# Attention in front of two expert layers: inputs laid out channel-major on the host, u products on TensorE, a new order of the attention loop

## What is computed

```python
batch, n_heads, seq, head_dim = (2, 8, 768, 48)
for t in range(S):
    kt, vt, rt, wt = (k[:, :, t], v[:, :, t], r[:, :, t], w[:, :, t])
    cur = np.einsum('bhd,bhe->bhde', u[None] * kt, vt)
    y[:, :, t] = np.einsum('bhd,bhde->bhe', rt, state + cur)
    state = wt[:, :, :, None] * state + np.einsum('bhd,bhe->bhde', kt, vt)
```

## Time and profile before

| | us |
|---|---|
| median of 3 runs | 1204.25 (1198.97 to 1204.97) |
| the profiled execution | 1201.32 |
| span of its profile | 1199.6 |
| TensorE busy | 1161.1 (97% of the span) |
| VectorE busy | 504.4 (42%) |
| ScalarE busy | 448.9 (37%) |
| GpSimd busy | 243.8 (20%) |

### The profile page before, as it was taken

One profiled execution on the slowest core, in us unless ns is written; L12 is line 12 of the kernel. 1 busy time (PEld: TensorE's weight loads), 2 busy tenths in 40 slices (PEclk: granted clock), 3 DMA queues, 4 the chain that ended last, 5 costly groups with the idle time before them and its releaser, 6 DMA issues. The chain is left out here.

```text
span 1199.6 us, 18556 instructions
## 1 busy us (share of the span) xinstructions
PE 1161.1 (97%) x6968; PEld 1039.6 (87%) x6968; DVE 504.4 (42%) x949; ACT 448.9 (37%) x926; POOL 243.8 (20%) x247
## 2 busy tenths in 40 slices
PE   6999989999999999999999999999999998999997
PEld 4888769899999998999999899999999986999997
DVE  5777556222222222212222222212222353999996
ACT  4565352212212211221221122122123473888884
POOL 5544262202201210220221121022012210000001
PEclk9888799999999999999999999999999999999999
DMA  9741043040050031005005002200300303999991
GB/s 187 144 70 31 2 149 124 26 160 1 1 186 1 1 132 55 1 2 185 1 1 185 1 1 91 94 1 1 105 1 1 132 35 114 392 358 368 359 361 59
DMA packets 106982, 123.41 MB, mean 103 GB/s; under 512 B 52745, under 2 KB 95406, under 8 KB 106912
## 3 DMA queue, kind: packets, MB, share of 16 engines
q1 hardware_dynamic: 104928, 117.65, 31.1%
q0 software_dynamic: 1984, 4.75, 1.0%
HBM read 98.37 MB, written 25.39 MB: 103 GB/s over the span
## 5 line engine op out<-in xcount | busy, mean ns | idle before, releaser
L973 DVE SCALAR_TENSOR_TENSOR h_lo<-hid,h_hi 128x512 fp32r<-128x512 f32 x168 | 116.1, 691 | 497.8 <-ACT h_hi L836 497.8
L836 ACT ACTIVATE h_hi<-hid 128x512 fp32r<-128x512 f32 x168 | 100.5, 598 | 547.7 <-PE hid L1131 547.7
L794 POOL TENSOR_TENSOR w_lo<-raw,w_hi 128x384 fp32r<-128x384 f32 x128 | 130.8, 1022 | 644.2 <-ACT w_hi L828 644.2
L1144 PE MATMUL acc<-w_hi,h_hi 128*128 128x384 f32 x736 | 249.6, 339 | 0.0
L1144 PE MATMUL acc<-w_hi,h_lo 128*128 128x384 f32 x736 | 249.3, 339 | 0.0
L1144 PE MATMUL acc<-w_lo,h_hi 128*128 128x384 f32 x736 | 248.6, 338 | 0.0
L1131 PE MATMUL hid<-x_hi,w_hi 128*128 128x512 f32 x576 | 227.9, 396 | 0.5 <-issue 0.4
L1131 PE MATMUL hid<-x_hi,w_lo 128*128 128x512 f32 x576 | 227.6, 395 | 0.0
L1131 PE MATMUL hid<-x_lo,w_hi 128*128 128x512 f32 x576 | 227.3, 395 | 0.0
L1144 PEld LDWEIGHTS acc<-w_lo,h_hi 128*128 128x128 f32 x736 | 138.1, 188 | 8.6
L1144 PEld LDWEIGHTS acc<-w_hi,h_hi 128*128 128x128 f32 x736 | 138.1, 188 | 7.7
(11 more groups left out here) (255 smaller groups left out, 1464.1 us busy)
## 6 DMA issues: line engine op xcount, KB each, us to landing
raw<-in_moe_w SPq DMA_DIRECT2D x54, 1536.0 KB, 9.2
rows<-filler SPq DMA_DIRECT2D x8, 2328.0 KB, 16.4
m_x<-rows SPq DMA_DIRECT2D x19, 194.0 KB, 4.6
spread_w<-in_w SPq DMA_DIRECT2D x16, 144.0 KB, 4.2
spread_r<-in_r SPq DMA_DIRECT2D x16, 144.0 KB, 4.1
spread_k<-in_k SPq DMA_DIRECT2D x16, 144.0 KB, 4.3
v_sb<-in_v SPq DMA_DIRECT2D x16, 144.0 KB, 4.2
out_y<-m_y,m_token POOLq DMA_INDIRECT x19, 6.7
```

The lines of the kernel that those rows point to most:

```text
L794: pool.tensor_tensor(lo[q][m][:, a:b], raw[m][:, a:b], hi[q][m][:, a:b].bitcast(F32), ALU.subtract).then_inc(s_wlo, 1)
L836: act.activation(h_hi[st % HB][:, :], hid[st % HB][:, :], ACT.Relu).then_inc(s_hhi, 1)
L973: dve.scalar_tensor_tensor(h_lo[st % HB][:, :], hid[st % HB][:, :], 0.0, h_hi[st % HB][:, :].bitcast(F32), ALU.max, ALU.subtract).then_inc ...
L1144: mm = pe.matmul(acc[j][:, 0:DM], a[st % HB][:, j * P:(j + 1) * P], b[q][1][:, f * DM:(f + 1) * DM], start=(f == 0 and x == 0), stop=(f == ...
```

## The change

r, k and w are laid out by the host (`laid_out`) as the channel-major tiles that the kernel used to make, with zeros (ones for w) in the padding, and v as v_sb holds it. So `spread`, the turn-ins and ScalarE's three copies go; `w_pad`, `k_ch` and `r_ch` are loaded directly, a DMA each (128 rows of 3 KB), v with one DMA too, and u as 96 columns of which two are not zero (`u_cols`).

The u term is one GpSimd product `rk` of 768 columns, then six TensorE products of `rk` with the 96 columns of `u_cols` (`sums`), and a small ScalarE copy to `cur`, which has two buffers. Behind the scores, `sums(j+1)` stands ahead of out_tiles(j,0) in TensorE's order. The copy and four state steps become one scan over all tiles (`carry` holds the factors, made by ScalarE in `carries`; increments are written with a stride of 5). Each score half has its own PSUM banks. The identity products are 240 columns wide, one ahead of turn_back and one between the score halves (four at the end as before).

The orders are new. VectorE: pre and suf of i+1, states(i), outputs(i-1,1), masked(i,0), products and keys of i+1, masked(i,1), receivers(i+1), outputs(i,0). The memsets of `state_diag` come behind the first two scans, and TensorE's first instructions wait for them.

```diff
+FIRST, BACK, MIDDLE, LAST = 5, 1, 1, 4
+WIDE = 96
...
             for i in range(PAIRS):
-                q = i % 2
-                for n in "wrk":
-                    if i >= 2:
-                        sp.wait_ge(s_turn[n], i - 1)
-                        if n != "w":
-                            sp.wait_ge(s_rk, i - 1)
-                    for h in two:
-                        sp.dma_start(spread[n][q][:, :, h, 0:D], src[n][i, h]).then_inc(s_in[n][q], 16)
+                if i >= 2:
+                    sp.wait_ge(s_suf, i - 1)
+                load(w_pad, w, "w", i)
+                if i >= 2:
+                    sp.wait_ge(s_kblk, i - 1)
+                    sp.wait_ge(s_rk, i - 1)
+                load(k_ch, k, "k", i)
+                if i >= 2:
+                    sp.wait_ge(s_rblk, i - 1)
+                load(r_ch, r, "r", i)
...
+            receiver_keys(0)
+            for j in range(PAIRS):
+                scaled(j)
+                if j + 1 < PAIRS:
+                    receiver_keys(j + 1)
+                current_values(j)
...
+            current(0)
+            for j in range(PAIRS):
+                divided(j, 0)
+                if j == 0:
+                    act.wait_ge(d_init, 6)
+                carries(j)
+                rows(j)
+                halves(j)
+                divided(j, 1)
+                diagonal(j)
+                if j + 1 < PAIRS:
+                    current(j + 1)
...
+                dve.tensor_tensor_scan(state[q][:, :, :].rearrange("p d t -> p (d t)"), carry[q][:, :, :].rearrange("p d t -> p (d t)"),
+                                       turn[:, 0:(NT - 1) * D], 0.0, ALU.mult, ALU.add).then_inc(s_state, 1)
...
+                if ahead:
+                    before_block(i + 1)
+                if ahead:
+                    behind_block(i + 1)
...
+                if back:
+                    states(i)
+                if i >= 1:
+                    outputs(i - 1, 1)
                 if back:
                     masked(i, 0)
                 if ahead:
-                    behind_block(i + 1)
                     products(i + 1)
                     keys(i + 1)
...
+            def sums(j):
+                pe.wait_ge(s_rk, j + 1)
+                if j == 0:
+                    pe.wait_ge(s_u, 16)
+                for t in range(NT):
+                    mm = pe.matmul(turn[:, CUR + 2 * t:CUR + 2 * t + WIDE], rk[:, t * P:(t + 1) * P], u_cols[:, j % (H // 2), :],
+                                   start=True, stop=True, skip_group_check=True)
+                mm.then_inc(s_sums, 1)
...
+            pe.wait_ge(d_init, 6)
+            for g in range(G):
+                for h in two:
+                    pe.matmul(score[g][h][:, 0:TG * P], ident[:, :], state_diag[0][:, 0:TG, :, :].rearrange("p n h c -> p (n h c)"),
+                              start=True, stop=True, skip_group_check=True)
+            sums(0)
+            for j in range(PAIRS):
+                pe.wait_ge(s_cur, j + 1)
+                keep_clock(FIRST if j == 0 else BACK)
+                turn_back(j)
+                if j >= 1:
+                    out_tiles(j - 1, 1)
+                increments(j)
+                scores(j, 0)
+                keep_clock(MIDDLE)
+                scores(j, 1)
+                if j + 1 < PAIRS:
+                    sums(j + 1)
+                out_tiles(j, 0)
+            keep_clock(LAST)
+            out_tiles(PAIRS - 1, 1)
```

More of the change, by code:

```diff
@@ L89, in attention @@
         k_rows = sb("k_rows", [P, NT, P])
-        state = [sb(f"state{q}", [P, NT, D]) for q in two]
+        state = [sb(f"state{q}", [P, D, NT - 1]) for q in two]
         state_diag = [sb(f"state_diag{q}", [P, NT, 2, 64]) for q in two]
-        rku = sb("rku", [P, NT, 2, D])
-        cur = sb("cur", [P, NT, 2])
+        carry = [sb(f"carry{q}", [P, D, NT - 1]) for q in two]
+        rk = sb("rk", [P, S])
+        cur = [sb(f"cur{q}", [P, NT, 2]) for q in two]
         cur_v = sb("cur_v", [P, NT, 2, D])
         scores_sb = [[sb(f"scores_sb{g}{h}", [P, TG, P]) for h in two] for g in range(G)]
-        turn_a = ps("turn_a", [P, 1024])
-        turn_b = ps("turn_b", [P, 1024])
-        score = [ps(f"score{h}", [P, 512]) for h in two]
+        turn = ps("turn", [P, 1024])
+        CUR, IDLE = S, S + 16
+        score = [[ps(f"score{g}{h}", [P, 512]) for h in two] for g in range(G)]
         yps = [ps(f"yps{g}", [P, 512]) for g in range(G)]
@@ L166, in _ @@
         def _(pool):
[L167 to L172, removed]
             def coef(c, at):
@@ L262, in rows, with halves @@
                     act.wait_ge(s_inc, j)
-                act.activation(flat(k_rows), turn_b[:, 0:S], ACT.Copy).then_inc(s_rows, 1)
-                divided(j, 1)
+                act.activation(flat(k_rows), turn[:, 0:S], ACT.Copy).then_inc(s_rows, 1)
+            def halves(j):
+                q = j % 2
+                act.wait_ge(s_rblk, j + 1)
+                if j >= 2:
+                    act.wait_ge(s_score, 4 * (j - 1))
+                act.activation(pairs_of(kr_half[q], BLK, HALF + BLK, 64), pairs_of(kr_blk[q], BLK, S + BLK, P), ACT.Copy).then_inc(s_half_a, 1)
             def diagonal(i):
@@ L271, in diagonal, with carries, current @@
                     act.activation(state_diag[i % 2][64 * h:64 * h + 64, 1:NT, h, 0:D],
[L272 to L282, removed]
+                                   state[i % 2][64 * h:64 * h + 64, :, :].rearrange("p d t -> p t d"), ACT.Copy).then_inc(s_diag, 1)
+            def carries(j):
+                act.wait_ge(s_kblk, j + 1)
+                if j >= 2:
+                    act.wait_ge(s_state, j - 1)
+                act.activation(carry[j % 2][:, :, 1:NT - 1], coef_r[:, 1:NT - 1, BT].unsqueeze(1).broadcast_to([P, D, NT - 2]),
+                               ACT.Copy).then_inc(s_carry, 1)
+            def current(j):
+                act.wait_ge(s_sums, j + 1)
+                if j >= 2:
+                    act.wait_ge(s_curv, j - 1)
+                act.activation(flat(cur[j % 2][:, :, :]), turn[:, CUR:CUR + NT * 2], ACT.Copy).then_inc(s_cur, 1)
+            current(0)
[10 more added lines that the diff above has]
+                    current(j + 1)
         @block.vector
@@ L386, in _ @@
                 back, ahead = i >= 0, i + 1 < PAIRS
+                if ahead:
+                    before_block(i + 1)
+                if ahead:
+                    behind_block(i + 1)
+                if i == -1:
+                    for q in two:
+                        dve.memset(carry[q][:, :, :], 0.0)
+                    for q in two:
+                        diag = dve.memset(state_diag[q][:, :, :, :], 0.0)
+                    diag.then_inc(d_init, 1)
                 if back:
                     states(i)
-                if ahead:
-                    before_block(i + 1)
+                if i >= 1:
+                    outputs(i - 1, 1)
                 if back:
@@ L440, in turn_back @@
                 for t in range(NT):
-                    mm = pe.transpose(turn_b[:, t * P:(t + 1) * P], k_tile[:, t * P:(t + 1) * P], ident[:, :])
+                    mm = pe.transpose(turn[:, t * P:(t + 1) * P], k_tile[:, t * P:(t + 1) * P], ident[:, :])
                 mm.then_inc(s_back, 1)
```

203 lines of the change are left out of this document (60 added, 143 removed).

## The result

The changed kernel takes 1172.48 us (median of four, 1169.51 to 1173.07), the kernel before 1201.61 beside it. The ratio is 0.976, with an interval of 0.973 to 0.980. Executions over 1.5% above the fastest of their kernel are left out of every ratio here, and are named where they occur. I had forecast 1179.5 in a range of 1170 to 1196: the time lies in the range, 7 us under the forecast and on the first rival (full clock, the lock binds: 1173).

The account below looks back on a forecast made before the run. Before, two legs in series set attention's 16.2 us period, no engine full; after, the VectorE/GpSimd lock and TensorE's clock would. Start 32.5 + 6 x 14.1 + end 11.4 = 128.5 us against 150.3, hence 1179.5 us, range 1170 to 1196.

Parts of the forecast that it names:

- first rival: Attention loop: TensorE stays at 2.4 GHz, the VectorE/GpSimd lock sets a 13.1 us period; 1173 us in all; chance 0.20.
- Where the time is: Whole kernel: expert layers, 1050 us at full clock, stay untouched; only attention, ending at 150.34 us, can move.
- Floor (b), the lock: Loop period: GpSimd's 6.8 us plus VectorE's 6.1 us of two-SBUF-input instructions exclude each other: 12.9 us, 13.3 with handovers.
- Floor (c), TensorE: Loop period: TensorE's own work per pair takes 11.5 us at full clock, 20.4 us at half clock.
- The clock: TensorE in the loop: half clock for 40% of the time, as before, giving a 13.9 us period, 14.1 with handovers.
- slower rival: Loop: clock stays at 0.61 without turn-ins, TensorE sets a 17.5 us period; 1209 us in all; chance 0.08.
- Start: Before the loop: first increments at 21.5 us instead of 24.47, those of pair 1 at 32.5 us.
- End: From the last increments to the end of attention: 11.4 us, against 12.6 before.
- The sum: Attention: 32.5 + 6 x 14.1 + 11.4 = 128.5 us against 150.3, 21.8 less; whole kernel 1179.5 us.
- The range: Whole kernel: 1170 to 1196 us, covering forecast, full clock and a third case, with 3 us for scatter.
- The case that I forecast: Attention loop: a period of 13.6 to 15 us, whole kernel 1175 to 1186 us; chance 0.45.
- The other signs: Trace of the loop: state scan near 0.6 us, sums 1.4 us with wait under 1 us, pair 7's increments near 117 us.

## Why the prediction was right, step by step

- *Where the time is.* Right: 30.3 of 31.8 us came out of attention.
- *Floor (b), the lock.* The mechanism and the order of the relay were right; the size was 13.3 for 12.43 us. The runs bear it out: 0.99 us more with a second r_tile, 0.5 us less with a short r x k. Laid beside the period above, k_tile ended at 1.6 (forecast 1.6), r product 2.4 (2.5), half 3.4 (3.4), `pre` 5.0 (5.2), r_tile 6.3 (6.7), `suf` 8.0 (8.4), r x k 9.6 (10.3), cur_v 10.7 (11.5), keys 12.4 (13.3). Each of the four that had been waiting (`pre`, r_tile, `suf`, r x k) came 0.1 to 0.2 us shorter behind the other than it is alone; I had added time at each handover.
- *Floor (c), TensorE.* 11.5 us at full clock: 11.58 where it is the bound. 20.4 at half clock: 20.09.
- *The clock.* This is the step that failed. "I see nothing that says which wins and take the same 40%" should have been 0% for eight of the eleven executions on record: 14.1 for 12.46 us in six periods is 9.8 us. The reading behind it was wrong as well: I took the one period of the kernel before that has no turn-ins (clock 0.61) as a sign that their loss costs the clock, and the changed kernel has none in any period and stands at 1.00. The slower rival's mechanism is real, but in other executions: at half clock TensorE is the bound, at 20.09 us a period in the changed kernel, 17.88 without identity products. What I missed is that the same kernel has two outcomes, 20 us apart, between which small things decide (identity products, the columns of the u products, waits of about 1 us); I took the mean of them. What the turn-ins had done for the clock no run tells.
- *Start.* 22.62 for 21.5: the four identity products took 5.49 us, I had 3.3 from a row at full clock. They are TensorE's first work, at 0.69 us a record (5.49 / 8) against 0.41 (1.65 / 4) in the kernel before, whose own first work, the six transposes at 6.68 us, took 1.51 us, as long as six turn-back records at half clock. The granted clock shows 1.00 in both places, so that half clock is inferred from the lengths alone. First period 11.4 for 11.0: together 1.5 us late (34.03 for 32.5). w landed just under 6 us, as taken.
- *End.* 11.2 for 11.4 us.
- *The sum.* 34.03 + 6 x 12.46 + 11.2 = 120.0, against 128.5: 8.5 us: 9.8 from the periods and 0.2 from the end, less 1.5 at the start. The execution profiled is 1.5 us shorter outside attention, which I can't place.
- *The range.* It held 1172.48 because it takes in the first rival, to which I gave 0.20; its lower end is 2.5 us away. The case that I forecast, a period of 13.6 to 15 us at a clock near 0.8, did not come. That the rival's 1173 is so near is partly luck: it had 13.1 for 12.46 us a period and 122.2 for 120.0, and the execution that the sum describes took 1169.51.
- *The other signs.* The state scan took 0.62 us (0.6), so the strided reads and PSUM writes cost nothing that shows; sums 1.41 us (1.4) behind a wait of 0.21; the increments of pair 7 came at 108.81 instead of near 117, which is the clock again.
- *The change, split.* Old order 14.25 us at full clock and 16.2 with its clock of 0.80; new order 12.43 at full clock. Seven periods: (14.25 - 12.3) x 7 = 14 us from the order and the work taken away, (16.2 - 14.25) x 7 = 14 us from the clock, the rest start and end. This is a reckoning and not a measurement: no run has the old order at full clock throughout, and its single periods of 14.25 us stand beside longer ones.

## What to carry to other kernels

Where TensorE's clock is below 1.00 in a stretch, work out its work per round at both levels before anything else: if the round at half clock is longer than the other engines' floor, the kernel can have two times, as this one has, and small things decide between them. A cheap dense product is worth a trial in such a loop where TensorE has a pause to put it in: it took 29 us off here and nothing off the kernel before. Each edit there needs several executions, not one. Between VectorE and GpSimd lay out the order in which they hand over the lock; ScalarE, whose twelve k_div pieces took 2.65 us in the kernel before and in this one whoever held the lock, is the place for a product that can be made in pieces.

## What I had not expected of the hardware

- TensorE at 1.2 GHz for some 105 us (45 to 150 us, without identity products in the loop) while busy all the time; full clock came back behind the four identity products at the end.
- Five falls of the clock in a loop in which TensorE did not pause (u products of 12 columns).
- The changed kernel, instruction for instruction the same, took 1168 to 1174 us or 1191.5 us.
- VectorE and GpSimd took turns at the lock in the full-clock periods read here, and an instruction that had been waiting for it was 0.1 to 0.2 us shorter from the handover than alone (r_tile 1.28 from 72.10 on, for 1.48).
